# Three of four experts stream the columns of x to TensorE in another order

## What is computed

```python
def _moe2_ref(x, domain_probs, w1, w2):       # x 3072 x 384, w1 4 x 384 x 1024, w2 4 x 1024 x 384
    p = domain_probs / (domain_probs.sum(-1, keepdims=True) + 1e-09)
    out = np.zeros((N, D), dtype=np.float32)
    for e in range(E):
        h = np.maximum(x @ w1[e], 0.0)
        out += p[:, e:e + 1] * (h @ w2[e])

x = attention(q, k, v, alpha)                 # state = alpha * state + k v^T, y = q state
x = (x @ w1) * (x @ w2) @ w3 @ w_out          # bilinear block, 384 -> 1024 -> 384
out = _moe2_ref(x, ...)
```

## Time and profile before

| | |
|---|---|
| median of 3 runs | 1219.95 us (1218.94 to 1220.34) |
| span of the profiled execution | 1217.6 us |
| TensorE busy, weight loads | 1212.3 us, 1118.6 us |
| VectorE, ScalarE, GpSimd busy | 461.4, 281.7, 168.8 us |
| up matmuls of the experts (L1175) | 1728 of 512 columns |
| down matmuls of the experts (L1294) | 2304 of 384 columns |

### The profile page before, as it was taken

How to read it: one execution, slowest core, us unless ns; L and a number is a source line. 1 busy time by engine, 2 the same in 40 slices (tenths; PEclk the granted TensorE clock), 3 DMA queues, 4 the chain that set the end, 5 groups by cost and what they waited for, 6 DMA issues and landing times.

```text
span 1217.6 us, 18865 instructions
## 1 busy us (share of the span) xinstructions
PE 1212.3 (100%) x7740; PEld 1118.6 (92%) x7740; DVE 461.4 (38%) x886; ACT 281.7 (23%) x526; POOL 168.8 (14%) x148
## 2 busy tenths in 40 slices
PE   9999999999999999999999999999999999999998
PEld 8799999999999999999999999999999999999998
DVE  6997586586651122122222222222122222222222
ACT  3443333333333311111111111111111111111111
POOL 1132222222223520000000000000000000000000
PEclk9999999999999999999999999999999999999999
DMA  9644444544415331100141111123101111222201
GB/s 286 207 121 122 126 132 106 137 128 105 126 47 195 106 145 52 51 17 36 53 156 52 52 52 52 52 73 135 42 15 46 52 52 53 78 78 78 78 9 44
DMA packets 87543, 108.03 MB, mean 89 GB/s; under 512 B 38576, under 2 KB 57904, under 8 KB 86960
## 3 DMA queue, kind: packets, MB, share of 16 engines
q1 hardware_dynamic: 87184, 106.63, 28.0%
q10 hardware_dynamic: 288, 0.39, 0.1%
HBM read 86.29 MB, written 18.35 MB: 86 GB/s over the span
## 4 chain that ended last, share of the span: by engine, by line
PE 99%; DVE 0%; issue 0%; DVEq 0%; ACT 0%
PE bank L1175 33%; PE bank L1294 25%; PE bank L1022 9%; PE bank L1024 9%; PE bank L1023 9%; PE score_banks L1294 8%; PE bank L1063 2%; PE bank L1244 1%; PE score_banks L1084 1%; PE bank L1073 1%; PE score_banks L1047 1%; PE bank L1226 1%; PE bank L1214 0%; DVE total L1000 0%; PE bank L1031 0%
## 5 line engine op out<-in xcount | busy, mean ns | idle before, releaser
L821 DVE SCALAR_TENSOR_TENSOR h_lo<-bank,h_hi 128x512 fp32r<-128x512 f32 x192 | 132.8, 691 | 584.9 <-ACT h_hi L601 584.0
L601 ACT ACTIVATE h_hi<-bank 128x512 fp32r<-128x512 f32 x192 | 114.7, 597 | 661.7 <-PE bank L1175 661.7
L1175 PE MATMUL bank<-x_hi,we_lo 128*128 128x512 f32 x576 | 228.7, 397 | 0.0
L1175 PE MATMUL bank<-x_hi,we_hi 128*128 128x512 f32 x576 | 224.1, 389 | 0.0
L1175 PE MATMUL bank<-x_lo,we_hi 128*128 128x512 f32 x576 | 223.5, 388 | 0.0
L1294 PE MATMUL bank<-we_hi,h_hi 128*128 128x384 f32 x576 | 194.6, 338 | 0.0
L1294 PE MATMUL bank<-we_lo,h_hi 128*128 128x384 f32 x576 | 194.5, 338 | 0.0
L1294 PE MATMUL bank<-we_hi,h_lo 128*128 128x384 f32 x576 | 193.8, 336 | 0.0
L499 POOL TENSOR_TENSOR we_lo<-we_raw,we_hi (+1 forms) x48 | 60.9, 1289 | 527.8 <-ACT we_hi L562 527.8
L1175 PEld LDWEIGHTS bank<-x_hi,we_lo 128*128 128x128 f32 x576 | 108.3, 188 | 22.4
L1175 PEld LDWEIGHTS bank<-x_lo,we_hi 128*128 128x128 f32 x576 | 108.0, 188 | 22.7
(11 more groups left out here) (99 smaller groups left out, 1473.3 us busy)
## 6 DMA issues: line engine op xcount, KB each, us to landing
x_hi<-x_hi_spill SPq DMA_DIRECT2D x24, 768.0 KB, 4.8
x_lo<-x_lo_spill SPq DMA_DIRECT2D x24, 768.0 KB, 6.3
we_raw<-wset SPq DMA_DIRECT2D x4, 3072.0 KB, 10.0
inputs<-akq SPq DMA_DIRECT2D x24, 448.0 KB, 5.2
values<-v_rows SPq DMA_DIRECT2D x24, 256.0 KB, 3.7
inputs<-akq SPq DMA_DIRECT2D x24, 224.0 KB, 3.3
x_hi_spill<-x_hi_out SPq DMA_DIRECT2D x8, 576.0 KB, 4.3
x_lo_spill<-x_lo_out SPq DMA_DIRECT2D x8, 576.0 KB, 5.2
```

Source lines behind the costliest of these rows:

```text
L601: act.activation(h_hi[:, s % 2, :], bank[s % 2][:, :], ACT.Relu).then_inc(h_hi_ready, 1)
L821: dve.scalar_tensor_tensor(out=h_lo[:, s % 2, :], in0=bank[s % 2][:, :], scalar=0.0, in1=h_hi[:, s % 2, :], op0=ALU.max, op1=ALU.subtract) ...
L1175: mm = pe.matmul(bank[s % 2][:, :], (we_hi if term < 2 else we_lo)[e % 2][:, cols], (x1_lo if term == 1 else x1_hi)[u][:, k, :], start=(i ...
```

## The change

In experts 1, 2 and 3 both patterns of an up matmul, the one that reads x1 and the one that writes the bank, go over the 512 columns in another order. The columns are seen as two halves of 256. From either half by turns come w columns in a row: w is 4 in expert 1, 2 in expert 2 and 8 in expert 3. Expert 0 keeps the plain order, and so does everything else.

```diff
+COLUMNS_AT_ONCE = [TILE2 // 2, 4, 2, 8]
...
                 cols = slice(k * FF + f * P, k * FF + (f + 1) * P)
-                mm = pe.matmul(bank[s % 2][:, :], (we_hi if term < 2 else we_lo)[e % 2][:, cols], (x1_lo if term == 1 else x1_hi)[u][:, k, :],
+                tokens, sums = (x1_lo if term == 1 else x1_hi)[u][:, k, :], bank[s % 2][:, :]
+                if e:
+                    tokens, sums = [a.rearrange("p (h c w) -> p c h w", h=2, w=COLUMNS_AT_ONCE[e]) for a in (tokens, sums)]
+                mm = pe.matmul(sums, (we_hi if term < 2 else we_lo)[e % 2][:, cols], tokens,
                                start=(i == 0), stop=(i == KT * TERMS - 1))
```

## The result

The changed kernel takes 1273.0 us (median of 4, 1272.51 to 1273.43) against 1219.45 us of the kernel before in the same series (1218.33 to 1220.34): a ratio of 1.044, 95% interval 1.0425 to 1.0454. It is slower by 53.6 us, where 93.7 us were forecast.

What follows compares the result with a forecast made beforehand. TensorE's matmuls were taken to bound the kernel; only expert 2's up stream was charged, 93.7 us on a 1217.6 us span, plus 2.35 us around it, giving 1313.6 us. Own range 1306 to 1320 us; 8-in-10 range 1217 to 1400 us.

Steps and rivals of the forecast that it cites:

- A: Rival: the new column order costs nothing and every step stays 4.16 us; 1220 us, chance 0.30.
- rival F: Expert 2 pays, but half, as other work absorbs part of the second piece: 46.9 us, 1267 us, chance 0.06.
- C: Rival: each run of columns has its own price, in read or write; 1307 or 1395 us, chance 0.18.
- expert 2 alone at half rate: Likeliest case: only expert 2's up matmuls fall to about half speed; 93.7 us extra, 1313.6 us, chance 0.32.
- The bound: Expert stage: TensorE is full and waits for nobody; time is the sum of what each matmul holds the array.
- Parts (1) and (2): Same instructions and weight loads; sums land in the same places, so ScalarE and VectorE are unchanged. Cost 0 each.
- part (3): Streams of the up matmuls in experts 1 to 3, the only term: from 0 to 217 ns extra per matmul.
- the float32 row: Plain float32 matmuls of L1244: 336 ns per 384 columns, 0.875 ns per column, about half the others' speed.
- the upper bound for expert 2: Expert 2's 432 up matmuls, in runs of two, each take 217 ns more than 231: 93.7 us.
- Experts 1 and 3 at 0: Up matmuls in runs of four and eight change 16-byte pieces as often as before, so 0 extra was taken.
- D: Rival: any jump breaks a prefetch, so experts 1 to 3 all fall to half rate; 281 us, 1501 us, chance 0.08.
- E: Rival: another address order misses collisions of moving read and weight load; at most 23 us faster, 1197 us, chance 0.06.

## Why the prediction was right in its direction and wrong in its size

The change is slower, as forecast, and 1273.0 us lies in the wide range of 1217 to 1400 us. But that range was wide because it had to take in rivals A, F and C. The likeliest case, expert 2 alone at half rate, had 1306 to 1320 us, and the time is outside of it. The nearest case was rival F (1267 us), which had a chance of 0.06 and another reason than the runs show.

- **The bound** held: TensorE's chain, nothing waited for, the clock at its upper level, and the loss is the sum of what each matmul holds the array. TensorE has 98% of the chain, not 99%, and the down matmuls of expert 2 take about 0.18 us, not 0.17. Parts (1) and (2) cost nothing, as said.
- **Both bounds** of part (3) were right: long runs with jumps cost nothing, and half rate exists; the single streams show 222 ns of extra, where 217 had been taken from the float32 row. That row was read a little high: the 336 ns are the mean of a piece of the chain, and inside it the starts lie 0.32 us apart (34.53 and 34.85 us in the timeline). That would be about 430 ns for 512 columns, and an up matmul of the single stream has 432 ns to the next start.
- **The step that failed is the choice of the upper bound for expert 2.** "runs of two need twice of it" counted a new piece for each run. But in the changed order a piece's second half is read when only one other run has passed since its first: of four runs two open a new piece and two come back to one that is at hand. The single stream of halves, where none comes back, pays 222 ns per matmul, and two places 256 columns apart of which none comes back pay 261 ns; the two halves by turns pay 101 ns; with four places the return seems to be too late, and the price is 273 ns. That a piece is kept is inferred from these prices: nothing in the trace shows it, and of the rules tried the last piece of each of two places fits best (two places 8 columns apart, and runs cut by a border of a piece). So the term was mis-sized, 43.7 us (0.91 x 48) for 93.7 us. My rival F had this size, 46.9 us, without this reason.
- **Experts 1 and 3 at 0** was nearly right: 0.12 and 0.10 us per step, 5.8 and 4.8 us, together 10.6, a fifth of the loss. The forecast had no term for them, and this part stays unexplained: it isn't a price per run (runs of 16 cost the most, runs of 64 nothing), and it shifts with distance and with the weight load.
- **The rivals.** A fell by expert 2. C wanted steps of 4.7, 5.2 and 4.4 us; expert 2 alone would nearly have fitted a price per run, expert 1 with half of the runs and an eighth of the price rules it out. D fell by experts 1 and 3. E forecast a gain, and none came: no tested order that reads each column once was faster. Its cause, collisions of the moving read with the weight load beneath, is only half tested: shortening the up matmuls' loads, which run beneath down matmuls, left the plain step at 4.17 us, but the down matmuls' loads, which run beneath the up matmuls, were left whole. A gain does exist, 11 ns per matmul, where 65 pieces serve all 512 columns. An order that reads each column once needs 128 pieces. So the excess may come from fetching new pieces; this is argued and not shown.
- **What the Trainium skill says of such patterns.** PSUM — Partial Sum Buffer, Specifications (TRN2), says that any non-contiguous pattern slows matmuls significantly. Advanced Engine Details and Errata, Memory Cachelines, has the same sentence, and next to it one that asks for every two consecutive elements to be contiguous in PSUM for best throughput. The trace disagrees with the first (0 ns for writes in runs of two, four and eight to two halves of a bank) and agrees with the second, as far as runs of two go; shorter ones were not tested. On the read side the trace agrees with that section's 16-byte lines in SBUF: what counts is the aligned piece of four columns. It does not agree with its "at least two hits" if a hit is one float32r column, since two columns of each line cost 222 ns extra; if a hit is a pair of columns it would fit, which no run here decides.

## What to carry to other kernels

Where float32r columns stream at about one per clock, as here, read the moving operand in whole, aligned pieces of four columns. A run of two by turns from two places, or a run of four begun in the middle of a piece, cost 96 to 116 ns on a matmul of 229, a stride or a stream of half pieces about twice the matmul's time. The exception is two places so near that both read the same pieces at once (4 columns apart: no price). An order that reads each column once and goes over each pair of neighbouring pieces that way was not tested. The sums may be written by turns to two halves of a bank, in runs of two, four or eight, at no cost, so a permutation of this kind that is wanted in the output belongs on the write side. A test of only one jumping pattern misleads in both directions: whether the other half of a piece is read soon sets more than half of the price.

## What the runs showed of the hardware that was not expected

- A single stream of two of each four columns, of every second, every third or every fourth column takes about the same, 220 to 236 ns more than 512 columns in plain order: about one column in two clocks, and skipping more hardly costs more.
- Places read by turns can be slower than half rate: 261 ns with two places and each run in a new piece, and with four and eight places, read and written, 273 and 312 ns of extra.
- The plain order isn't the fastest possible stream. Re-reading neighbouring pieces gave a step of 4.06 us, an up matmul about 217 ns against 229 from start to start, near the 213 ns of 512 clocks at 2.4 GHz.
